# Attention with a relative-position bias, then two mixtures of experts: the bias stage and the attention in one program block

## The chip, the cores and the metric

The program runs on one core of one Trainium2 chip. The metric is the device time of one execution in microseconds (us), from start to end, with the inputs already in device memory. TensorE is called PE here, VectorE DVE, ScalarE ACT, GpSimd POOL and SyncE SP, as the profile does.

## The reference, cut to what matters

```python
# attention: q, k, v are [4, 8, 576, 64] (batch, heads, seq, dim)
scores = scale * q @ k^T
psi_rel = log1p(|i - j|);  psi_i = log1p(max(i, 1))
h = max((psi_rel / psi_i)[..., None] @ w1 + b1, 0)     # w1 [1, 32], b1 [32]
bias = h @ w2                                          # w2 [32, 8]: one 576x576 table a head
attn = softmax(scores + bias);  out = attn @ v
# then x [2304, 512] = out, heads side by side
# mixture 1: gate, softmax, one expert of 8 a token, h = relu(x @ w1[e]), h @ w2[e], times the gate
# mixture 2: h = max(x @ w1, x @ w2, x @ w3);  out = h @ w_out
```

All is float32. The change touches only the bias tables and the start of the attention. The two mixtures are as they were.

## The kernel before, in words

The kernel has three program blocks one after another, and each block has a stream of instructions for each engine. A block ends for all engines together.

**Bias stage** (`build_bias`, L53). It makes the eight 576x576 tables and stores them in device memory (`bias_table`, [row, head, column]). A step makes 16 rows for all heads. There are 36 steps, run as loops of 12 turns with 3 steps each (L148, L182, L124), with addresses from registers. In a step DVE makes three of four hidden tiles of 128x576 (L154, multiply and maximum) and ACT the fourth (L166, Relu). PE sums them with a block-diagonal w2 (L205, 8 matmuls of 288 columns into two banks), ACT evacuates the sums with a constant added (L174), and SP stores the result (L128, 288 KB). Hidden tiles, sums and evacuated tiles each have a ring of three. DVE's tiles for step s therefore wait for the sums of step s-3. ACT's evacuation of step s waits for the store of step s-3. On ACT the hidden tile of step s+2 stands ahead of the evacuation of step s.

Ahead of the loops SP issues the table of log distances (L116), w1 and b1 (L118) and four copies of w2 (L122). All of these raise one semaphore, `loaded`, for which DVE and PE wait. Then SP issues an identity and, for both units of head 0, the keys and queries (L443, L371, L372). ACT waits for DVE's `base` and then loads its function table. POOL sets some tiles to zero and issues 24 small loads for the later routing (L1072).

**Attention** (`build_attention`, L211). Eight heads, two units a head (a unit is two batches), five steps a unit. Ahead of the loop over heads the first unit is prepared, as a chain from engine to engine. PE transposes the keys and queries of unit (0, 0) (L652). ACT rounds them to the near part (L852, L854), and DVE makes the rest (L737, L738). PE transposes the 64 remaining rows (L669), DVE splits them (L746, L748), and POOL places them (L532, L534). Then PE makes the first scores (L598), DVE adds the bias and finds the maximum (L727), and ACT takes the exponential (L832). Here SP waits for all 36 stores, then loads the bias rows of head 0 (five tiles, L478 to L482), the values of both units (L406, L408) and the keys of head 1. In a step of the loop PE makes the scores of the next step, turns the probabilities of this one (L638), and multiplies them with the values of the unit before (L623).

**Mixtures** (`build_moe`, L1091): most of the time, untouched by the change.

The order in each engine's stream is written out by hand in the code. No planner sets it.

Of the kernel before, what the change touches and what calls it, by code (L numbers as in the profile page):

```python
# [16 lines left out]
ALU = mybir.AluOpType  # L17
# [35 lines left out]
def build_bias(nc, w1, b1, w2, bias_dram, stored, space, meanwhile_sync, meanwhile_gpsimd):  # L53
# [3 lines left out]

    G = P // HIDDEN
    ROWS = G * G
    STEPS = SEQ // ROWS
    WIN = 2 * SEQ - 1 - (G - 1)
    RING = len(stored)
# [12 lines left out]
    with ExitStack() as ctx:  # L78
        def sb(name, shape, dt=F32):
            return ctx.enter_context(nc.sbuf_tensor(name, shape, dt))  # L80

        def sem(name):
            return ctx.enter_context(nc.semaphore(name))

        both = sb("both", [P, WIN + SEQ // G])
        win, rows = both[:, 0:WIN], both[:, WIN:]
        scale = sb("scale", [P, SEQ // G])
        w1c = sb("w1c", [P, 1])
        b1c = sb("b1c", [P, 1])
        nb1 = sb("nb1", [P, 1])  # L90
        w2bd = sb("w2bd", [P, G * HEADS])
        hid = nc.alloc_sbuf_tensor_at("hid", [P, RING, G, SEQ], F32, offset=space)
        base = sb("base", [P, 1])
        staged = nc.alloc_sbuf_tensor_at("staged", [P, RING, SEQ], F32, offset=space + 4 * RING * G * SEQ)
        acc = ctx.enter_context(nc.psum_tensor("acc", [P, RING, 2, BANK], F32))
        cacc = ctx.enter_context(nc.psum_tensor("cacc", [P, BANK], F32))

        zeroed = sem("bias_zeroed")
        loaded = sem("bias_loaded")
        scales_done = sem("bias_scales_done")  # L100
        const_mm = sem("bias_const_mm")
        base_zeroed = sem("bias_base_zeroed")
        base_done = sem("bias_base_done")

        hid_dve = [sem(f"hidden_by_dve{r}") for r in range(RING)]
        hid_act = [sem(f"hidden_by_act{r}") for r in range(RING)]
        summed = [sem(f"bias_summed{r}") for r in range(RING)]
        evacuated = [sem(f"bias_evacuated{r}") for r in range(RING)]
        block = ctx.enter_context(nc.Block())
        rows_per_step = bias_dram.rearrange("(s r) h j -> s (r h) j", r=ROWS)  # L110
        TURNS = STEPS // RING
        LOADS = 16 * (3 + G)

        @block.sync
        def _(sp):
            sp.dma_start(both[:], tables_dram).then_inc(loaded, 16)  # L116
            for dst, src in ((w1c, w1), (b1c, b1.rearrange("(a k) -> a k", a=1))):
                sp.dma_start(dst[:], src.rearrange("a k -> k a").unsqueeze(0).broadcast_to([G, HIDDEN, 1])).then_inc(loaded, 16)  # L118

            sp.wait_ge(zeroed, 1)  # L120
            for g in range(G):
                sp.dma_start(w2bd[g * HIDDEN:(g + 1) * HIDDEN, g * HEADS:(g + 1) * HEADS], w2).then_inc(loaded, 16)  # L122
            meanwhile_sync(sp)
            with sp.Fori(0, TURNS) as t:  # L124
                for r in range(RING):

                    sp.wait_ge(evacuated[r], t + 1)
                    sp.dma_start(rows_per_step[bass.ds(t * RING + r, 1)].rearrange("a p j -> (a p) j"),  # L128
                                 staged[:, r, :]).then_inc(stored[r], 16)

        @block.gpsimd
        def _(pool):
            meanwhile_gpsimd(pool)

        @block.vector
        def _(dve):
            nc.vector.memset(w2bd[:], 0.0).then_inc(zeroed, 1)
            nc.vector.memset(base[:], 0.0).then_inc(base_zeroed, 1)
            dve.wait_ge(loaded, LOADS)
            nc.vector.tensor_scalar(nb1[:], b1c[:], -1.0, None, ALU.mult).then_inc(scales_done, 1)  # L140
            nc.vector.tensor_scalar(scale[:], rows, w1c[:], None, ALU.mult).then_inc(scales_done, 1)

            dve.wait_ge(const_mm, 1)
            dve.wait_ge(base_zeroed, 1)
            nc.vector.tensor_copy(base[0:DVE_Q * HIDDEN, :], cacc[0:DVE_Q * HIDDEN, 0:1]).then_inc(base_done, 1)
            dve.wait_ge(scales_done, 2)

            with dve.Fori(0, TURNS) as t:  # L148
                for r in range(RING):

                    dve.wait_ge(summed[r], t)
                    for q in range(DVE_Q):
                        u = (t * RING + r) * G + q
                        last = nc.vector.tensor_scalar(  # L154
                            hid[:, r, q, :], win[:, bass.ds(-G * u + (SEQ - G), SEQ)], scale[:, bass.ds(u, 1)],
                            nb1[:], ALU.mult, ALU.max)
                    last.then_inc(hid_dve[r], 1)

        @block.scalar
        def _(act):  # L160
            def hidden(t, r):

                act.wait_ge(summed[r], t)
                for q in range(DVE_Q, G):
                    u = (t * RING + r) * G + q
                    last = nc.scalar.activation(hid[:, r, q, :], win[:, bass.ds(-G * u + (SEQ - G), SEQ)], ACT.Relu,  # L166
                                                bias=b1c[:], scale=scale[:, bass.ds(u, 1)])
                last.then_inc(hid_act[r], 1)

            def evacuate(t, r):  # L170

                act.wait_ge(summed[r], t + 1)
                act.wait_ge(stored[r], 16 * t)
                nc.scalar.activation(staged[:, r, :].rearrange("p (a j) -> p a j", a=2), acc[:, r, :, 0:HALF],  # L174
                                     ACT.Identity, bias=base[:]).then_inc(evacuated[r], 1)

            act.wait_ge(scales_done, 2)
            act.wait_ge(base_done, 1)

            for r in range(RING - 1):  # L180
                hidden(0, r)
            with act.Fori(0, TURNS - 1) as t:  # L182
                for r in range(RING):
                    ahead = r + RING - 1
                    hidden(t + ahead // RING, ahead % RING)
                    evacuate(t, r)
            hidden(TURNS - 1, RING - 1)
            for r in range(RING):
                evacuate(TURNS - 1, r)

        @block.tensor
        def _(pe):
            pe.wait_ge(loaded, LOADS)
            for q in range(DVE_Q):
                last = nc.tensor.matmul(cacc[q * HIDDEN:(q + 1) * HIDDEN, 0:1], w2bd[:], b1c[:], start=True, stop=True)
            last.then_inc(const_mm, 1)
            with pe.Fori(0, TURNS) as t:
                for r in range(RING):

                    pe.wait_ge(hid_dve[r], t + 1)  # L200
# [1802 lines left out]
```

## Time and profile before

| what | value |
|---|---|
| median of 3 runs | 1037.75 us (1036.89 to 1039.24) |
| profiled execution, own time | 1038.5 us |
| its span | 1036.9 us |
| granted PE clock, mean | 0.981 |
| PE busy | 961.4 us, 93% of the span |
| DVE / ACT / POOL busy | 530.9 / 392.2 / 283.4 us |
| largest groups of PE | L1612 193.2, L1533 145.7, L1567 140.3, L638 80.7, L598 69.3 us |

The profile is of one execution. Its span runs from the first to the last instruction, and 1.6 us of its own time lie around it. Matmuls are pipelined, so a busy PE isn't PE at its peak. A time in the span is counted from its start: the bias stage fills the first 67 us, the attention reaches to about 370 us. An idle stretch of an engine is put down to what ended it.

### The profile page before, as it was taken

How to read it: one execution, taken by the hardware profiler on the slowest of the kernel's cores; microseconds unless marked ns; L12 is line 12 of the kernel's file. 1: busy time of each engine (PE TensorE's matmuls, PEld its weight loads, DVE VectorE, ACT ScalarE, POOL GpSimd, SP SyncE). 2: the span in 40 equal slices, each digit the busy share in tenths (PEclk: the TensorE clock that was granted, in tenths of full speed). 3: DMA queues.
4: the chain of work that ended last, by engine and by line, in shares of the span. 5: the costliest groups of instructions: out<-in, count | busy, mean ns of one | idle time of the engine just before them, and what ended most of it. 6: DMA issues, size and time to landing. Idle time of an engine off the chain costs nothing.

```text
span 1036.9 us, 19507 instructions
## 1 busy us (share of the span) xinstructions
PE 961.4 (93%) x6432; PEld 790.2 (76%) x6432; DVE 530.9 (51%) x1066; ACT 392.2 (38%) x810; POOL 283.4 (27%) x310
## 2 busy tenths in 40 slices
PE   4869999999999974799999999999999999999998
PEld 1227677677676663688888888888989999999997
DVE  6966666667566548444444457444352323333331
ACT  5967777777777652242100024034311010111100
POOL 5014150010101035796300059268531010100100
PEclk9989999999999996899999999999999999999999
DMA  7565544454443256775300036246411010100001
GB/s 168 203 205 133 128 125 110 110 119 106 100 114 85 76 163 205 237 211 172 104 21 21 22 122 210 84 131 186 132 51 41 21 41 21 41 21 11 21 11 31
DMA packets 125746, 106.68 MB, mean 103 GB/s; under 512 B 88073, under 2 KB 91305, under 8 KB 125689
## 3 DMA queue, kind: packets, MB, share of 16 engines
q1 hardware_dynamic: 86600, 56.27, 19.3%
q10 hardware_dynamic: 33632, 34.02, 11.6%
q0 software_dynamic: 5456, 15.60, 4.8%
q8 instruction: 40, 0.66, 0.3%
q14 instruction: 18, 0.14, 0.0%
HBM read 79.24 MB, written 26.61 MB: 102 GB/s over the span
## 4 chain that ended last, share of the span: by engine, by line
PE 56%; POOL 3%; issue 2%; DMA 1%; DVE 1%; ACT 1%; ACTq 0%; POOLq 0%
PE moe_banks L1612 19%; PE moe_banks L1533 12%; PE moe_banks L1567 12%; PE moe_banks L1629 7%; POOL slots L1301 3%; PE moe_banks L1551 2%; PE moe_banks L1518 1%; DMA x_tok<-in_moe_w_out 1%; PE moe_banks L1470 1%; PE moe_banks L1595 1%; PE moe_banks L1479 0%; DMA x_behind<-x_rows_by_tile,source 0%; POOL far_weights L1301 0%; ACT x_tok L1431 0%; POOL x_tok L1339 0%
## 5 line engine op out<-in xcount | busy, mean ns | idle before, releaser
L1612 PE MATMUL moe_banks<-yT,slots 128*128 128x384 f32 x1080 | 193.2, 334 | 0.7 <-ACT best L1439 0.7
L1612 PEld LDWEIGHTS moe_banks<-yT,slots 128*128 128x128 f32 x1080 | 187.9, 188 | 1.5 <-ACT best L1439 1.0
L1301 POOL TENSOR_TENSOR slots<-x_tok,slots 128x512 fp32r<-128x512 f32 (+1 forms) x116 | 140.9, 1249 | 155.3 <-ACT slots L1409 154.9
L1409 ACT CAST slots<-x_tok 128x512 fp32r<-128x512 f32 (+1 forms) x116 | 67.9, 602 | 261.9 <-PE moe_banks L1533 128.1
L1533 PE MATMUL moe_banks<-slots,xT 128*128 x600 | 145.7, 399 | 1.2 <-issue 1.2
L1567 PE MATMUL moe_banks<-slots,hT 128*128 x600 | 140.3, 389 | 0.8 <-POOL slots L1301 0.8
L727 DVE CUSTOM_DVE_ANT_0 probs<-s_ps,bias 128x576 f32<-128x576 f32 x144 | 103.7, 754 | 71.0 <-PE s_ps L598 51.4
L1533 PEld LDWEIGHTS moe_banks<-slots,xT 128*128 128x128 f32 x600 | 112.6, 191 | 25.0 <-issue 1.9
L1567 PEld LDWEIGHTS moe_banks<-slots,hT 128*128 128x128 f32 x600 | 112.6, 188 | 24.4 <-issue 1.1
L832 ACT ACTIVATE probs<-probs,negmax 128x576 f32<-128x576 f32 x144 | 110.6, 771 | 22.3 <-DVE negmax L727 21.6
L1867 DVE TENSOR_TENSOR best<-best,moe_banks 128x384 f32<-128x384 f32 x36 | 19.9, 554 | 132.8 <-PE moe_banks L1612 127.5
L840 ACT COPY pT<-t_ps 128x512 f32<-128x512 f32 x112 | 64.9, 581 | 60.4 <-PE t_ps L638 60.3
L638 PE MATMUL t_ps<-ident,probs 128*128 128x128 f32 x576 | 80.7, 281 | 3.7 <-ACT probs L832 1.1
L598 PE MATMUL s_ps<-kT,qT 64*128 64x288 f32 x768 | 69.3, 313 | 11.7 <-DVE negmax L727 9.0
L1629 PE MATMUL moe_banks<-wo,u 128*128 128x512 f32 x324 | 76.5, 393 | 0.0
L638 PEld LDWEIGHTS t_ps<-ident,probs 128*128 128x128 f32 x576 | 63.2, 142 | 16.0 <-issue 9.5
L598 PEld LDWEIGHTS s_ps<-kT,qT 64*128 64x128 f32 x768 | 54.4, 189 | 27.1 <-issue 15.3
L1439 ACT COPY best<-moe_banks 128x384 f32<-128x384 f32 x33 | 15.8, 478 | 152.4 <-PE moe_banks L1612 152.4
L623 PE MATMUL o_ps<-pT,v_raw 128*64 128x288 f32 x512 | 72.5, 415 | 0.7 <-ACT out_T L859 0.5
L1629 PEld LDWEIGHTS moe_banks<-wo,u 128*128 128x128 f32 x324 | 60.1, 188 | 12.2
L1347 POOL DMA_INDIRECT out<-o,out_row_of x15 | 14.7, 982 | 198.2 <-ACT o L1446 198.2
L532 POOL TENSOR_TENSOR kT<-last_T,one 128x128 fp32r<-128x128 f32 x32 | 14.6, 457 | 198.1 <-DVE last_T L748 198.1
(199 smaller groups left out, 1186.9 us busy)
## 6 DMA issues: line engine op xcount, KB each, us to landing
x_tok<-in_moe_w ACTq DMA_DIRECT2D x96, 256.0 KB
bias_table<-staged SPq DMA_DIRECT2D x36, 288.0 KB, 2.1
bias<-bias_table SPq DMA_DIRECT2D x32, 288.0 KB, 2.7
result_rows<-y SPq DMA_DIRECT2D x25, 256.0 KB, 2.0
x_tok<-in_moe_w ACTq DMA_DIRECT2D x24, 192.0 KB
k_raw<-in_k SPq DMA_DIRECT2D x32, 128.0 KB, 2.4
q_raw<-in_q SPq DMA_DIRECT2D x32, 128.0 KB, 2.5
v_raw<-in_v SPq DMA_DIRECT2D x32, 128.0 KB, 2.3
```

What stands on the lines that cost most here:

```text
L598: last = nc.tensor.matmul(s_ps[:, slot, half, 0:HALF], qT[u][a][lanes, s * P:(s + 1) * P], keys[c][lanes, at:at + HALF], start=(n == 0), s ...
L623: last = nc.tensor.matmul(o_ps[b * DH:(b + 1) * DH, 0:HALF], v_raw[u][:, b, jb, :], moving, start=(jb == 0), stop=(jb == FULL))
L638: last = nc.tensor.transpose(t_ps[:, bank, jb * P:(jb + 1) * P], probs[:, slot, at:at + P], ident[:])
L727: nc.vector.tensor_tensor_reduce(probs[:, step, b * SEQ:(b + 1) * SEQ].rearrange("p (a j) -> p a j", a=2), s_ps[:, slot, :, 0:HALF], bias[ ...
L832: nc.scalar.activation(row, row, ACT.Exp, bias=negmax[:, 2 * step + b:2 * step + b + 1], scale=-1.0, accum_out=sums[:, u, tile:tile + 1]). ...
L840: nc.scalar.copy(*turned_probs(u, s, b, bank)).then_inc(emptied[bank], 1)
L1301: nc.gpsimd.tensor_tensor(rest, raw(n, rows), near.bitcast(F32), ALU.subtract).then_inc(part_done(e, part)[0], 1)
L1409: nc.scalar.copy(near, raw(n, rows)).then_inc(near_done, 1)
L1533: return nc.tensor.matmul(h_ps[:, side, :], xT[t % 2][:, a, d * P:(d + 1) * P], weights(parity, b, d * FF + side * BANK), start=first, sto ...
L1567: last = nc.tensor.matmul(y_ps, hT[:, a, f * P:(f + 1) * P], weights(parity, b, 2 * PER_W + f * MODEL), start=(f == 0 and n == 0), stop=(f ...
L1612: last = nc.tensor.matmul(u_ps[m], final_weight(far, slots, m, d, a, f), yT[:, c, d, :], start=(d == 0 and k == 0), stop=(d == KD - 1 and ...
L1629: last = nc.tensor.matmul(o_ps[j], u[:, c, f, j * P:(j + 1) * P], wo[:, a, f, :], start=(f == 0 and k == 0), stop=(f == KF2 - 1 and k == 2))
```

## The change

The bias stage becomes four functions, one for each engine but POOL, that are called inside the attention's block. The loops become 36 steps written out, with constant addresses. After a step each engine runs a hook, `after_step`, in which parts of the attention's start are placed. The ring semaphores become counts over all steps.

- SP: w2's four copies are now issued by ACT. After the first loads SP issues the identity and the keys and queries of unit (0, 0), those of unit (0, 1) after the store of step 4, the values of unit (0, 0) after step 20 and of unit (0, 1) after step 22. Bias tiles 0 to 3 of head 0 are loaded after steps 9, 17, 25 and 33, the last after step 35.
- POOL: the routing loads wait for `loaded`. Its split work (L532, L534) follows in the same stream.
- ACT: one unused Relu of 128x1 ahead of the steps, so that the function table is loaded there. The near parts come after the evacuations of steps 10 and 11.
- DVE: the rests after steps 13 and 14, the last rows after step 19.
- PE: keys and queries turned after step 8, the last rows after step 16, the first scores after step 33. Sums go to the attention's own banks: in turn s_ps[0], s_ps[1] and the joined r_ps/o_ps, and the last three steps to t_ps, r_ps/o_ps, t_ps. PE waits for all 36 evacuations before it turns the first probabilities.

```diff
-def build_bias(nc, w1, b1, w2, bias_dram, stored, space, meanwhile_sync, meanwhile_gpsimd):
+def bias_stage(nc, sb, sem, w1, b1, w2, bias_dram, stored, space, banks, first_bank):
...
+    def sync(sp, after_step):
+        sp.dma_start(both[:], tables_dram).then_inc(loaded, 16)
+        for dst, src in ((w1c, w1), (b1c, b1.rearrange("(a k) -> a k", a=1))):
...
+        after_step(sp, -1)
+        for s in range(STEPS):
+            sp.wait_ge(evacuated, s + 1)
+            sp.dma_start(rows_per_step[s], staged[:, s % RING, :]).then_inc(stored[s % RING], 16)
+            after_step(sp, s)
...
+    def scalar(act, after_step):
+        act.wait_ge(zeroed, 1)
+        for g in range(G):
+            act.dma_start(w2bd[g * HIDDEN:(g + 1) * HIDDEN, g * HEADS:(g + 1) * HEADS], w2).then_inc(loaded, 16)
+        act.wait_ge(base_zeroed, 1)
+        nc.scalar.activation(unused[:], base[:], ACT.Relu).then_inc(base_zeroed, 1)
...
+            act.wait_ge(summed, s + 1)
+            if s >= RING:
+                act.wait_ge(stored[s % RING], 16 * (s // RING))
...
         def first_split(pool):
...
+            pool.wait_ge(*bias_sems["loaded"])
             routing["load"](pool)
...
+        LAST_SUMS = {BIAS_STEPS - 3: t_ps, BIAS_STEPS - 2: ro_ps, BIAS_STEPS - 1: t_ps}
...
+        TURN_AT, NEAR_AT, REST_AT, TURN_LAST_AT, LAST_AT = 8, (10, 11), (13, 14), 16, 19
+        SCORES_AT = BIAS_STEPS - 3
...
+            def after_step(sp, s):
+                if s == -1:
+                    sp.dma_start(ident[:], identity_dram).then_inc(ident_in, 16)
+                    keys_queries(sp, 0, 0)
+                if s == 4:
+                    keys_queries(sp, 0, 1)
+                if s == 20:
+                    sp.wait_ge(zeroed, 1)
+                    load_values(sp, 0, 0)
+                if s == 22:
+                    load_values(sp, 0, 1)
+                steps = s - 1
+                if steps > 0 and steps % (P // BIAS_ROWS) == 0 or s == BIAS_STEPS - 1:
+                    steps = SEQ // BIAS_ROWS if s == BIAS_STEPS - 1 else steps
+                    for r in range(BIAS_RING):
+                        sp.wait_ge(bias_stored[r], 16 * stored_by(r, steps))
+                    bias_tile(0, (steps - 1) // (P // BIAS_ROWS))
...
+                        if first and u == 0 and s == 0:
+                            pe.wait_ge(bias_sems["evacuated"], BIAS_STEPS)
...
+            def after_step(pe, s):
+                if s == TURN_AT:
+                    pe.wait_ge(ident_in, 16)
+                    pe.wait_ge(bias_sems["base_done"], 1)
+                    for g in (KEYS, QUERIES):
+                        bank, count = prologue_fill(g)
+                        turn_rows(0, 0, g, t_ps[:, bank]).then_inc(filled[bank], 1)
+                if s == TURN_LAST_AT:
+                    prepare_last(0, 0, prologue_fill(LAST))
+                if s == SCORES_AT:
+                    pe.wait_ge(zeroed, 1)
+                    pe.wait_ge(bias_sems["evacuated"], SCORES_AT - 1)
+                    scores(0, 0, 0, [prologue_fill(QUERIES)])
```

## Rows read from the trace of the kernel before

**Rows 1.** Stretches: busy us of each engine (count), granted PE clock, DMA share, GB/s.
```profile
15.00:50.00 35.00, 28.46 (x392) 10.36 (x388) 35.00 (x73) 34.72 (x49) 0.00 (x0) 1.00 0.53 200
70.65:74.85 4.20, 1.81 (x12) 1.46 (x12) 0.32 (x1) 0.00 (x0) 3.95 (x11) 0.50 0.99 310
72.40:80.00 7.60, 5.69 (x34) 5.02 (x35) 2.89 (x8) 2.62 (x6) 2.24 (x7) 0.50 0.73 183
80.00:92.00 12.00, 10.82 (x92) 8.52 (x90) 8.64 (x21) 9.94 (x24) 1.70 (x4) 0.99 0.60 141
```

**Rows 2.** Timeline, 0 to 60 us: start, us, engine, line, [idle before <-releaser].
```profile
1.98 0.56 SPq L118 DMA_DIRECT2D b1c<-in_b  x1
2.58 1.86 SPq L122 DMA_DIRECT2D w2bd<-in_w  x4
...
3.34 10.87 POOL L1072 DMA_DIRECT2D mod_id<-in_moe_modality_id  x20
...
9.60 0.59 SPq L371 DMA_DIRECT2D k_raw<-in_k  x1
9.82 0.15 DVE L140 TENSOR_SCALAR nb<-b1c 128x1 f32<-128x1 f32 x1 [8.90 <-DMA w2bd<-in_w]
...
10.46 1.28 ACT L166 ACT_TABLE_LOAD   x1 [10.46 <-DVE base L145]
...
10.85 49.46 DVE L154 TENSOR_SCALAR hid<-both,scale,nb 128x576 f32 x100 [0.48 <-DVE scale L141]
...
13.79 0.52 SPq L372 DMA_DIRECT2D rem_raw<-in_q  x1
...
24.70 0.75 ACT L174 ACTIVATE staged<-acc,base 128x576 f32<-128x576 f32 x1
...
26.08 0.75 ACT L174 ACTIVATE staged<-acc,base 128x576 f32<-128x576 f32 x1
```

**Rows 3.** DMA issues of 0 to 120 us: kind, count, KB each, median us to landing.
```profile
bias_table<-staged SPq DMA_DIRECT2D x36, 288.0 KB, 2.1
...
mod_id<-in_moe_modality_id POOLq DMA_DIRECT2D x16, 1.0 KB, 3.5
```

**Rows 4.** Timeline, 59 to 100 us: the end of the bias stage.
```profile
58.76 5.47 DVE L154 TENSOR_SCALAR hid<-both,scale,nb 128x576 f32 x11
...
61.77 0.86 ACT L166 ACTIVATE hid<-both,b1c,scale 128x576 f32<-128x576 f32 x1
...
64.29 1.18 PE L205 MATMUL acc<-hid,w2bd 128*32 128x288 f32 x16 [0.29 <-DVE hid L154]
65.54 0.74 ACT L174 ACTIVATE staged<-acc,base 128x576 f32<-128x576 f32 x1 [0.73 <-PE acc L205]
```

**Rows 5.** The same timeline: from the new block to the second exponential.
```profile
67.22 0.35 POOL L551 MEMSET own_batch<- 64x64 f32 x2 [52.25 <-POOLq L78]
...
68.69 0.69 DVE L737 TENSOR_TENSOR kT<-t_ps,kT 128x512 fp32r<-128x512 f32 x1 [4.46 <-ACT kT L852]
...
69.90 0.28 DVE L746 CAST last_T<-t_ps 128x128 fp32r<-128x128 f32 x1
...
74.53 0.76 DVE L727 CUSTOM_DVE_ANT_0 probs<-s_ps,bias 128x576 f32<-128x576 f32 x1 [4.03 <-PE s_ps L598]
...
75.33 0.78 ACT L832 ACTIVATE probs<-probs,negmax 128x576 f32<-128x576 f32 x1 [6.17 <-DVE negmax L727]
...
79.49 0.78 ACT L832 ACTIVATE probs<-probs,negmax 128x576 f32<-128x576 f32 x1
```

**Rows 6.** Instructions of L154, all, then of 12.8 to 15.3 us: ns min/median/max.
```profile
L154 DVE TENSOR_SCALAR hid<-both,scale,nb x108: 561/573/833, 10.9 to 63.7; 128x576 f32 x108
...
L154 DVE TENSOR_SCALAR hid<-both,scale,nb x6: 561/605/833, 12.3 to 15.2; 128x576 f32 x6
```

**Rows 7.** Timeline of POOL, then of DVE, around 753 us, and L1874's instructions.
```profile
750.10 6.81 POOL L1358 TENSOR_TENSOR wo<-x_tok,wo 128x3072 fp32r<-128x3072 f32 x1 [8.97 <-ACT wo L1455]
...
753.44 3.70 DVE L1874 CAST u<-best 128x384 fp32r<-128x384 f32 x1
...
L1874 DVE CAST u<-best x36: 359/359/3697, 733.6 to 1021.3; 128x384 fp32r<-128x384 f32 x36
```

More of the change, by code:

```diff
@@ L76, in build_bias @@
     tables_dram = nc.inline_tensor(np.ascontiguousarray(tables), name="bias_tables").ap()
[L78 to L193, printed above, removed]
-            for q in range(DVE_Q):
[L195 to L200, printed above, removed]
-                    pe.wait_ge(hid_act[r], t + 1)
-                    pe.wait_ge(evacuated[r], t)
-                    for a in range(2):
-                        for q in range(G):
-                            last = nc.tensor.matmul(acc[q * HIDDEN:(q + 1) * HIDDEN, r, a, 0:HALF], w2bd[:],
-                                                    hid[:, r, q, a * HALF:(a + 1) * HALF], start=True, stop=True)
-                    last.then_inc(summed[r], 1)
@@ new lines, in scalar, with hidden, evacuate @@
+    def scalar(act, after_step):
[4 more added lines that the diff above has]
+        nc.scalar.activation(unused[:], base[:], ACT.Relu).then_inc(base_zeroed, 1)
+        def hidden(s):
+            if s >= RING:
+                act.wait_ge(summed, s - RING + 1)
+            for q in range(DVE_Q, G):
+                u = s * G + q
+                last = nc.scalar.activation(hid[:, s % RING, q, :], window(u), ACT.Relu, bias=b1c[:], scale=scale[:, u:u + 1])
+            last.then_inc(hid_act, 1)
+        def evacuate(s):
+            act.wait_ge(summed, s + 1)
+            if s >= RING:
+                act.wait_ge(stored[s % RING], 16 * (s // RING))
+            nc.scalar.activation(staged[:, s % RING, :].rearrange("p (a j) -> p a j", a=2), banks(s)[:, :, 0:HALF],
+                                 ACT.Identity, bias=base[:]).then_inc(evacuated, 1)
+        act.wait_ge(scales_done, 2)
+        act.wait_ge(base_done, 1)
+        for s in range(RING - 1):
+            hidden(s)
+        for s in range(STEPS):
+            if s + RING - 1 < STEPS:
+                hidden(s + RING - 1)
+            evacuate(s)
+            after_step(act, s)
@@ new lines, in tensor @@
+    def tensor(pe, before_step, after_step):
+        pe.wait_ge(loaded, LOADS)
+        for q in range(DVE_Q):
+            last = nc.tensor.matmul(first_bank[q * HIDDEN:(q + 1) * HIDDEN, 0:1], w2bd[:], b1c[:], start=True, stop=True)
+        last.then_inc(const_mm, 1)
+        for s in range(STEPS):
+            pe.wait_ge(hid_dve, s + 1)
+            pe.wait_ge(hid_act, s + 1)
+            before_step(pe, s)
+            for a in range(2):
+                for q in range(G):
+                    last = nc.tensor.matmul(banks(s)[q * HIDDEN:(q + 1) * HIDDEN, a, 0:HALF], w2bd[:],
+                                            hid[:, s % RING, q, a * HALF:(a + 1) * HALF], start=True, stop=True)
+            last.then_inc(summed, 1)
+            after_step(pe, s)
@@ L490, in values_rows @@
+            bias_sync(sp, after_step)
             def values_rows(it):
```

140 lines of the change are left out of this document (92 added, 48 removed).

## The prediction

> **What bounds the kernel now.** I read the stretches first, then the timeline of the first 100 us. In 15 to 50 us DVE is busy for all 35.00 us, PE for 28.5, at full clock [rows 1]: DVE bounds the bias stage. Its first hidden tile starts at 10.85 and the last ends at 58.76 + 5.47 = 64.23 [rows 2, 4]. That is 53.38 us for 108 tiles, 0.494 each and 1.48 a step, without a gap. Then comes the hand-over: the last sums start at 64.29, the last evacuation at 65.54 [rows 4], the new block at 67.22, the first bias addition at 74.53, the first exponential at 75.33 and that of the second step at 79.49 [rows 5]. From DVE's last tile to the first exponential are 11.1 us in which PE runs its few matmuls at a granted 0.50, and it keeps that level, 1.2 GHz, to 80 us. From 80 on it has 0.99, 2.4 GHz [rows 1]. After that the attention runs as a steady chain, in which nothing is tied to the start of the program, only to what came before. So what moves the second exponential moves the end by as much. I follow that one point.
>
> **Part 1, the loads ahead of the stage.** DVE starts at 9.82, released by w2's copies. SP issues these from 2.58 to 4.44, behind b1, while POOL issues its loads from before 3.34 [rows 2]. In the new order ACT issues the copies beside SP's first loads, and POOL's loads wait for `loaded`. The last needed issue is then b1's, from 1.98 on. Its landing under a full queue isn't shown. From below it is the 2.1 us of a store, from above the whole 9.82. The nearest row is POOL's small loads in the same microseconds, 3.5 us [rows 3], which gives 1.98 + 0.56 + 3.5 = 6.0. I take 6.1 (4.6 to 9.8): 3.7 us earlier. DVE's first hidden tile stays 1.03 behind it (10.85 - 9.82), at 7.1. ACT's table load of 1.28 goes from after `base` to this wait. It lay beside DVE's first tiles, so it brings nothing on DVE's path, only ACT starts level with DVE.
>
> **Part 2, steps written out.** The register instructions of the loops run on the sequencers while the tiles run, and DVE has no gap [rows 1, 2]. I take 0 for their going. If an address cost DVE anything, the gain would be up to 0.03 a tile, 3 us. The nearest row, a stage without any gap, says 0.
>
> **Part 3, DVE's moved work.** The rests of keys and queries start 0.61 after each other, and the last rows take from 69.90 to the start of POOL's part at about 70.65, with two waits of DVE for itself: 0.8. Sum 2 x 0.61 + 0.8 = 2.0 us [rows 1, 5]. DVE is the bound, so all is on the path. 7.1 + 53.4 + 2.0 = 62.5.
>
> **Part 4, what SP does between the stores.** The keys and queries of unit (0, 1) are eight issues. In the trace such a group goes from 9.60 to 14.31, 4.7 us [rows 2]. After step 4's store they stand ahead of step 5's store. That one lands 0.4 + 4.7 + 2.1 = 7.2 us after step 4's evacuation ends, and 8.2 if the queue holds it up by 1 us beside the small packets. ACT's evacuation of step 8 needs it. ACT would be there after 4 x 1.38 - 0.62 = 4.9 us (24.70 to 26.08 is a step at ACT's own pace [rows 2]). So ACT is 3.3 us late. The two near copies after steps 10 and 11 add 1.2. Of these 4.5 us some are covered. ACT's hidden tile is ahead of DVE's: the last one ends at 62.6, 1.6 before DVE's [rows 4], and I take 1.0 at step 8. The ring lets DVE go on for 1.6 more: it needs sums of 65.5 only two steps after its tiles [rows 4]. Left are 1.9 us (0.7 to 3.4). The other moved loads, values of 2.2 us after steps 20 and 22 and bias tiles of 0.9, are shorter than the ring's 4.4 us less a landing of 2.1. I take 0. Likewise PE's nine transposes: PE has 35.0 - 28.5 free in 35 us [rows 1], 0.3 a step. 64.4.
>
> **Part 5, POOL's work beside DVE.** The splitting and the routing bias, 3.95 us in 11 instructions [rows 1], and two memsets of 0.35 [rows 5] ran while DVE stood nearly still. Now they run beside the hidden tiles. The trace has one clear place for this: POOL's subtraction runs from 750.10 to 756.91, and a DVE cast from SBUF to SBUF, which takes 359 ns elsewhere, starts at 753.44 and ends at 757.14, just behind it [rows 7]. DVE stood still until POOL was done. The hidden tiles are of that sort: 576 columns in 0.494 us, while 512 columns out of PSUM take 0.69 [rows 5, 6]. Bounds: 0 if the two interleave, 4.3 if each POOL instruction stops DVE for its length. I take 3.3, three quarters, as POOL waits for itself in between. POOL's descriptor writing costs less: the six tiles beside its last loads have a median of 605 ns against 573, and one has 833 [rows 6]. Over a longer stretch, early, partly inside the stall of part 4: 0.3. Together 3.6: DVE's last tile ends at 68.0.
> The Trainium skill says in "GPSIMD Engine Reference", section "Key points", that POOL shares its SBUF interfaces with DVE and contends with DVE instructions in a two-port mode or with two SBUF inputs. "VectorE: DVE Perf Modes", section "Mode 2×_2P", counts a float32 multiply by a scalar from SBUF to SBUF into that mode. By that rule the place where POOL's work was, beside an idle DVE, was the good one, and the change gives up to 4.3 us back. Without the rule the same sum would come out 3.6 us lower.
>
> **Part 6, the new hand-over.** Bias addition and first scores are ready: DVE adds right behind its last tile, 0.76 for the first half. ACT is last. Sums start 0.06 after DVE's end, evacuation 1.25 later, and it holds ACT for 0.63 [rows 4]. The score matmuls after step 33, about 1.1 us at full clock, exceed PE's free time of the last two steps by 0.2. So the first exponential comes 2.1 behind DVE: 70.1, against 75.33. The next step also comes sooner: in the trace 79.49 - 75.33 = 4.2 us, with PE at 0.50 and scores only begun behind the exponential. With PE at full clock and the second scores made while ACT still evacuates, what is left is two exponentials of 0.77 and the copy of the first probabilities, about 2.3 us: 1.9 less (1.0 to 2.3). What is late next is that copy.
>
> **Sum.** 75.33 - 70.1 = 5.2, plus 1.9: 7.1 us. Against the profiled execution: span 1036.9 - 7.1 = 1029.8, own time 1038.5 - 7.1 = 1031.4. The median of the runs shown lies 0.75 below that execution, so I predict 1037.75 - 7.1 = 1030.6.
>
> **The rivals.** *A, POOL and DVE don't hinder each other.* For it: the tiles beside POOL's loads are only 32 ns longer in the median [rows 6]. Against: rows 7. It gives 3.6 more: 1027.0. If the loads also end at 5 us, 1026.
> *B, the loads come no sooner.* `loaded` has seven parts, and the keys of unit (0, 0) are now issued 2 us earlier, beside them. For it: loads alone fill the queues to 0.99 in 70.65 to 74.85 [rows 1]. Against: POOL's loads are gone. It costs the 3.7 of part 1: 1034.3.
> *C, slower: the ring of stores decides every step.* An evacuation waits for the store three steps back. Three steps are 4.4 us, of which evacuation and issue take about 1, so from a landing of 3.4 to 3.5 us on the ring sets the pace, and each further us costs 36 / 3 = 12 us. The stage now loads about 2.6 MB of keys, values and bias rows between its stores. Stores land in 2.1 us at a DMA share of 0.53 [rows 1, 3]. For a loss the landing would have to be over 4.1 us all along. At 4.6 the time is 1030.6 + 13 = 1044. It speaks against it that the extra bytes are a quarter of the stores' 10.4 MB (36 x 288 KB) and come in seven short bursts.
> *D, the time comes back later.* Were the attention paced by weight loads or POOL's early chunks, nothing would reach the end: 1037.8. But these are issued behind the same chain.
>
> **How the numbers follow.** Forecast 0.60, with its own range 1028.3 to 1033.0 (part 4 at either end, part 1 a microsecond or so to either side). A 0.20, B 0.13, C 0.03, D 0.04. The range reaches to A and to B: 1026.3 to 1034.5. Beyond it lie C, D and a joint of the worst parts. About 0.2% (2 us) is what a measurement of this kernel can tell from no change. Faster 0.93 (forecast, A, B), the same 0.04 (D), slower 0.03 (C).
>
> **What would show it.** `loaded` near 6 us and DVE's first tile near 7. A gap of DVE of about 2 us around steps 12 to 15, ended by PE, with ACT's evacuation of step 8 released by a store. Tiles of DVE of 0.8 to 1 us beside POOL's placing, around 40 to 50 us, 573 ns elsewhere. The first exponential near 70 and the second step's 2.3 later, PE at 1.00 throughout. From there to the end the length as before, within 1 us. I am wrong if DVE's tiles are longer throughout, if DVE waits for PE in most steps (C), or if the stretch from the second exponential to the end changes.

## The result and the profile after

| | runs | median us | range |
|---|---|---|---|
| before | 4 | 1037.49 | 1036.89 to 1039.24 |
| after | 4 | 1026.55 | 1024.52 to 1028.92 |

The ratio is 0.9893, with an interval of 0.9868 to 0.9917: 10.9 us faster. Forecast were 1030.6 us and a gain of 7.1. The direction and the place were right, the size fell short by nearly 4 us: 1026.55 lies below the forecast's own range (1028.3 to 1033.0) and 0.25 us inside the wide one, which reached that far for rival A. The profiled execution of the kernel after took 1028.92 us, its span is 1027.1.

The busy times of the page: TensorE still fills nearly the whole span.

```profile
PE 962.7 (94%) x6432; PEld 791.8 (77%) x6432; DVE 532.9 (52%) x1066; ACT 391.0 (38%) x811; POOL 286.0 (28%) x310
...
bias_table<-staged SPq DMA_DIRECT2D x36, 288.0 KB, 2.4
```

The timeline of the kernel after, from its start to the second exponential (columns as in [rows 2]); it answers to [rows 2, 4, 5]:

```profile
0.93 1.81 ACTq L131 DMA_DIRECT2D w2bd<-in_w  x4
...
6.17 0.15 DVE L112 TENSOR_SCALAR nb<-b1c 128x1 f32<-128x1 f32 x1 [5.26 <-DMA w2bd<-in_w]
...
6.60 21.93 DVE L124 TENSOR_SCALAR hid<-both,scale,nb 128x576 f32<-128x576 f32 x42
...
8.38 10.71 POOL L1098 DMA_DIRECT2D mod_id<-in_moe_modality_id  x20
...
20.00 0.74 ACT L147 ACTIVATE staged<-s_ps,base 128x576 f32<-128x576 f32 x1 [1.04 <-DMA bias_table<-staged]
...
22.34 4.93 SPq L105 DMA_DIRECT2D bias_table<-staged  x5
...
24.79 0.74 ACT L147 ACTIVATE staged<-ro_ps,base 128x576 f32<-128x576 f32 x1 [1.91 <-DMA bias_table<-staged]
...
28.81 0.69 DVE L754 TENSOR_TENSOR kT<-t_ps,kT 128x512 fp32r<-128x512 f32 x1 [0.28 <-ACT kT L874]
...
39.59 24.66 DVE L124 TENSOR_SCALAR hid<-both,scale,nb 128x576 f32<-128x576 f32 x48 [0.15 <-DVE last_T L765]
...
40.04 0.67 POOL L527 TENSOR_TENSOR qz<-last_T,own_batch 128x128 fp32r<-128x128 f32 x1
...
64.17 0.74 DVE L744 CUSTOM_DVE_ANT_0 probs<-s_ps,bias 128x576 f32<-128x576 f32 x1
...
65.95 0.74 ACT L147 ACTIVATE staged<-t_ps,base 128x576 f32<-128x576 f32 x1 [0.50 <-PE t_ps L171]
66.58 0.77 ACT L854 ACTIVATE probs<-probs,negmax 128x576 f32<-128x576 f32 x1
...
68.73 0.78 ACT L854 ACTIVATE probs<-probs,negmax 128x576 f32<-128x576 f32 x1
```

Three distances are to be read here. DVE's first hidden tile starts at 6.60, 4.25 us sooner than before. Its last ends at 39.59 + 24.66 = 64.25, the same place as the 64.23 of before: the moved work and POOL's work have used up the earlier start. From there to the first exponential it is 2.33 us instead of 11.1, and to the second 4.48 instead of 15.3. So the second exponential comes 79.49 - 68.73 = 10.76 us sooner.

The stretches of the kernel after (columns as in [rows 1]):

```profile
15.00:50.00 35.00, 25.76 (x353) 10.21 (x349) 34.53 (x69) 31.02 (x45) 11.74 (x22) 1.00 0.71 228
66.58:68.73 2.15, 1.32 (x14) 0.91 (x11) 1.44 (x4) 2.10 (x6) 0.00 (x0) 1.00 0.37 129
...
362.00:366.00 4.00, 4.00 (x21) 4.00 (x20) 1.86 (x3) 2.24 (x5) 3.02 (x3) 0.52 0.20 66
```

DVE is still the full engine of the bias stage, POOL now works 11.74 us beside it, and at the hand-over TensorE keeps its full 2.4 GHz, where it had 0.50 before, from 70.65 to 80 us [rows 1]. The last row lies at the other end of the attention, where the mixtures begin. There 32 transposes come first. TensorE's timeline in the kernel before, after, and before once more:

```profile
371.68 3.69 PE L1470 MATMUL moe_banks<-ident_late,x_tok 128*128 128x128 f32 x32 [2.00 <-PEq L221]
```
```profile
359.80 6.64 PE L1496 MATMUL moe_banks<-ident_late,x_tok 128*128 128x128 f32 x32 [2.00 <-PEq L194]
```
```profile
372.10 6.59 PE L1470 MATMUL moe_banks<-ident_late,x_tok 128*128 128x128 f32 x32 [2.00 <-PEq L221]
```

The attention ends 371.68 - 359.80 = 11.88 us sooner. The profiled spans differ by only 9.8, since in the execution after the clock fell to 0.52 for a part of the transposes, which cost 2.95. The kernel before does the same in its second profile. A third length, 5.0 to 5.35 us, is found in most of the other profiles. So it comes with either kernel. The same holds of a wait of TensorE some 40 to 50 us on: 9.04 us before and 8.01 after in this first pair, 4.7 to 7.0 in the four profiles of the third group of experiments, and 1.3 to 1.6 in the eight of the first two groups, the second one of the kernel before among them. It goes with the group, and so with the chip or the time, and not with the change. So I measure the change at the start of the mixtures where one trace stands for a kernel, and by medians where there are several runs.

### The profile page after: what moved, and what is told of

Same layout as the page of the kernel before. It is cut to its first block, busy times and chain, and to the rows that moved or that the text cites. A ratio compares the mean times of both kernels' runs of the same rounds, so it can differ in the third digit from the quotient of the medians.

```text
span 1027.1 us, 18990 instructions
## 1 busy us (share of the span) xinstructions
PE 962.7 (94%) x6432; PEld 791.8 (77%) x6432; DVE 532.9 (52%) x1066; ACT 391.0 (38%) x811; POOL 286.0 (28%) x310
## 4 chain that ended last, share of the span: by engine, by line
PE 59%; POOL 2%; DVE 2%; issue 1%; ACT 0%; ACTq 0%
PE moe_banks L1638 22%; PE moe_banks L1559 13%; PE moe_banks L1593 12%; PE moe_banks L1655 7%; PE moe_banks L1577 2%; POOL slots L1327 2%; PE moe_banks L1496 1%; PE moe_banks L1544 1%; PE moe_banks L1621 1%; PE moe_banks L1505 0%; DVE slots L1802 0%; POOL x_tok L1365 0%; DVE in_lane L1740 0%; ACT x_tok L1457 0%; ACT slots L1435 0%
## 5 line engine op out<-in xcount | busy, mean ns | idle before, releaser
L617 PE MATMUL ro_ps<-pT,v_raw 128*64 128x288 f32 x512 | 72.5, 415 | 0.7 <-ACT out_T L881 0.5
```

The costliest lines, as they stand in the source:

```text
L617: last = nc.tensor.matmul(o_ps[b * DH:(b + 1) * DH, 0:HALF], v_raw[u][:, b, jb, :], moving, start=(jb == 0), stop=(jb == FULL))
```

## The experiments

All are compared with runs of the kernel before on the same chip: median 1035.52 us (22 runs) in the first group of four, 1035.12 (9 runs) in the second group, 1036.9 (one run) in the third.

### The same kernel again (after_again)

No edit.

> The changed kernel once more, beside the kernel before. Theory 1 (the change is worth 10.8 us at the second step's exponential and 11.9 us at the end of the attention; the 3.0 us lost behind it in the first profile are a matter of the moment at which PE's clock is lowered): here the second step's exponential starts again at 68.7 us, and the 32 first transposes of the mixtures take either 3.7 or up to 6.7 us, with the span longer or shorter by just that. Theory 2 (the change itself causes the slow transposes): they take 6.6 us again. Time 1025 to 1029 us, 0.9875 to 0.991 of before.

Measured: 1023.14 us, ratio 0.9882 (0.9866 to 0.9898). First hidden tile 7.07, last one's end near 64.9, second exponential 69.19, the first 32 transposes 5.24. Of the gain of 12.4 us 11.4 to 11.8 are there at the start of the mixtures (360.32 against 371.68 and 372.10). The first profile's 2.95 us extra at these transposes were 1.55 here (5.24 - 3.69), so their length isn't fixed by the kernel.

### One block, but the preparation behind the stage (prep_behind)

The main lines of the edit:

```
-        TURN_AT, NEAR_AT, REST_AT, TURN_LAST_AT, LAST_AT = 8, (10, 11), (13, 14), 16, 19
-        SCORES_AT = BIAS_STEPS - 3
+        TURN_AT, TURN_LAST_AT, LAST_AT, SCORES_AT = [BIAS_STEPS - 1] * 4
```

> One block, steps written out, loads as in the changed kernel, but the first unit's preparation (turning, rounding, splitting, placing, first scores) stands behind step 35 on every engine. Theory 1 (most of the hand-over's 11.1 us was the preparation as a chain, the end of the block only about 1.5 us of it): DVE's last tile ends about 2.3 us sooner than in the changed kernel (near 62), the first exponential comes about 8 to 9 us behind it (near 71) and the second step's near 75, so 6 us of the gain are lost: 1032 to 1033 us. Theory 2 (the barrier between the blocks was the main cost): the first exponential near 68 and 1028 us.

Measured: 1033.19 us, ratio 0.9975 (0.9966 to 0.9984). Timeline of DVE and ACT at the hand-over:

```profile
62.08 1.56 DVE L124 TENSOR_SCALAR hid<-both,scale,nb 128x576 f32<-128x576 f32 x3 [0.45 <-PE ro_ps L171]
69.03 0.69 DVE L749 TENSOR_TENSOR kT<-t_ps,kT 128x512 fp32r<-128x512 f32 x1 [5.40 <-ACT kT L868]
...
75.00 0.76 DVE L739 CUSTOM_DVE_ANT_0 probs<-s_ps,bias 128x576 f32<-128x576 f32 x1 [4.15 <-PE s_ps L591]
...
66.91 0.74 ACT L147 ACTIVATE staged<-t_ps,base 128x576 f32<-128x576 f32 x1 [0.65 <-PE t_ps L171]
...
75.80 0.77 ACT L848 ACTIVATE probs<-probs,negmax 128x576 f32<-128x576 f32 x1 [6.30 <-DVE negmax L739]
...
79.97 0.78 ACT L848 ACTIVATE probs<-probs,negmax 128x576 f32<-128x576 f32 x1
```

The two exponentials come at 75.80 and 79.97, where the kernel before has them at 75.33 and 79.49. My expectation, 71 and 75, was wrong. The earlier loads gave 4.3 us at the front. But DVE waits for the ring: it stands behind step 13 for 1.0 us and behind steps 29, 31 and 34 for 0.4 to 0.6, each time until TensorE has made sums, while ACT waits for stores six times in this stage, 5.8 us in all. With POOL's loads beside it the stage takes 57.07 us and not 53.38, and its last tile ends only 0.6 us sooner. The last sums start 2.0 us behind that tile, 0.06 in the kernel before [rows 4]. From there the preparation runs one engine after the other as in the kernel before, with TensorE at 0.50 from 72 to 80 us.

The end of the block has a price of its own, which this run hides behind those late sums. From the end of ACT's last evacuation to the first transpose it is 1.13 us in the kernel before (65.54 + 0.74 to 67.41) and 0.10 here (66.91 + 0.74 to 67.75). TensorE's timeline, before and in this run:

```profile
67.41 0.63 PE L652 MATMUL t_ps<-ident,k_raw 128*128 128x128 f32 x4 [1.94 <-PEq L78]
```
```profile
67.75 0.63 PE L645 MATMUL t_ps<-ident,k_raw 128*128 128x128 f32 x4 [0.90 <-issue]
```

So one block and the early loads alone bring the second exponential no sooner. The 10.8 us there need the preparation to lie beside the stage, and the early loads pay for its room.

### The kernel before with its steps written out (steps_written_out)

The four loops over the turns of the ring become Python loops, nothing else. One of them:

```
-            with dve.Fori(0, TURNS) as t:
+            for t in range(TURNS):
```

> The kernel before with nothing changed but its four loops of the bias stage, which are written out with constant addresses. Theory 1 (register instructions are hidden, as predicted): DVE's tiles start 0.489 us after each other as before, first tile 0.2 to 0.4 us sooner as no registers are set up, time within 0.5 us of before (1037). Theory 2 (addresses from registers cost DVE up to 0.03 us a tile): 3 us faster.

Measured: 1032.40 us, ratio 0.9972 (0.9961 to 0.9982). The tiles start 0.489 us after each other as before, so within the stage the forecast of nothing holds. Yet the kernel is 3.1 us faster, a miss. The trace shows 1.1 to 1.5 us of it at the attention's end (its last exponential starts at 358.69, against 359.79 and 360.21): 0.4 to 0.7 are there by the second exponential, the rest is a head loop of 36.07 us a head instead of 36.20. The remainder lies behind the start of the mixtures, where executions differ anyway. But the 3.1 us stand between medians of 11 and 22 runs, and the interval is clear of 1. prep_behind, whose steps are written out too, looks the same: 2.3 us faster by medians, with its second exponential no sooner and the mixtures only 0.4 to 0.9 us sooner (371.25 against 371.68 and 372.10). So of the whole change's 12.4 us in after_again up to 3 may come from writing the steps out, and only 1.1 to 1.5 of these are seen in a trace. The kernel before wasn't profiled in this group, so where the rest lies isn't settled.

### POOL's routing loads and routing bias later (pool_all_later)

```
-            pool.wait_ge(*bias_sems["loaded"])
-            routing["load"](pool)
...
+            place_last(0, 1)
+            routing["load"](pool)
             token_bias(pool)
-            place_last(0, 1)
```

> The changed kernel with POOL's routing loads and routing bias behind the placing of unit (0, 1), so that in the bias stage POOL only places unit (0, 0). Theory 1 (POOL's work makes the hidden tiles beside it longer, by 1.3 us in all beside its descriptor writing and 1.1 us beside its elementwise work, but the first part hides a wait of DVE for ACT's near copy, which is late by the stores): no tile of DVE over 0.50 us except four beside the placing, DVE waits about 1.6 us for the near copy at step 13 in place of 0.3, and its last tile ends 0.8 us sooner (63.4); time 0.5 to 1 us below the changed kernel. Theory 2 (ACT isn't late enough to matter): the tile ends 2.1 us sooner, at 62.1, and the time is 2 us lower.

Measured: 1023.66 us, ratio 0.9891 (0.9869 to 0.9914): as the kernel after. DVE's tiles are back at 0.489 from the start and only the placing stretches some, by 0.73 us in all. 42 tiles take 20.64 us where they took 21.93, so POOL's loads had cost 1.3. The last tile ends at 63.48, as expected. The gain to the first exponential is 0.9 us (65.67). Head 0 then takes 34.85 us instead of 32.95 and gives 1.9 back. DVE's timeline shows why it brought so little, a wait that had been 0.28:

```profile
28.47 0.69 DVE L753 TENSOR_TENSOR kT<-t_ps,kT 128x512 fp32r<-128x512 f32 x1 [1.29 <-ACT kT L873]
```

### The kernel before again (before_again)

No edit.

> The kernel before, profiled beside the others. Theory 1 (the wait of 8 to 9 us some 40 us into the mixtures, seen in both first profiles and in none of the second series, belongs to the chip or the moment and not to a kernel): it isn't there, and the span from the end of the attention is 660 to 662 us as in the second series; the second step's exponential starts at 79.5 us and a head of the attention's loop takes 36.20 us. Theory 2 (the kernels with written-out steps lose that wait by themselves): it is there.

Measured: 1036.37 us. Second exponential 79.84, heads of 36.20, first transposes 6.59, and 1.3 us where the first profile had its 9.04. The attention's numbers repeat to 0.4 us, the mixtures' first 50 us don't.

### Second unit's keys and queries ahead of the stage (keys_up_front)

```
                 if s == -1:
                     sp.dma_start(ident[:], identity_dram).then_inc(ident_in, 16)
                     keys_queries(sp, 0, 0)
-                if s == 4:
                     keys_queries(sp, 0, 1)
```

> The changed kernel with the keys and queries of unit (0, 1) issued right behind those of unit (0, 0), not between the stores of steps 4 and 5. Theory 1 (the late stores cost 0.3 to 0.6 us only, because POOL's work had slowed DVE's tiles by then): ACT waits for no store at steps 8, 10 or 11, DVE doesn't wait for the near copy at step 13, and DVE's last tile ends 0.3 to 0.6 us sooner, at 63.7; time within 1 us of the changed kernel. Theory 2 (as predicted, the stores cost 1.9 us): it ends at 62.3 and the time is 2 us lower.

Measured: 1021.15 us, ratio 0.9868 (0.985 to 0.9885). SP has no eight issues between two stores any more, the wait at step 13 is gone, and DVE's last tile ends near 63.85, as the first theory expected. ACT still waits for stores twice, 1.4 us in all, where it had four times and 5.0. `loaded` is there at 6.23, within the 6.10 to 6.64 of the other profiles with these first loads and POOL's behind them. Second exponential 68.20. The kernel after has no runs in this group. Against the kernel before of its group this one gains 14.0 us where after_again gained 12.4, and the two intervals overlap.

### Routing loads and bias behind head 2 (routing_after_head2)

The two calls of pool_all_later, put behind the written-out heads, ahead of the loop over heads.

> The changed kernel with POOL's routing loads and routing bias behind head 2's placing, where POOL has nothing else. Theory 1: DVE's last tile ends at 63.5 as with the same work behind unit (0, 1), and now the 1.9 us that were lost there in head 0 (unit (1, 0) placed late) are kept: the ninth step's exponentials and all later ones 1.0 us ahead of the changed kernel, time 1 us lower. Theory 2 (POOL's loads disturb DVE wherever they are): the gain is lost again within the attention.

Measured: 1023.51 us, ratio 0.9886 (0.9866 to 0.9905). Head 0 loses nothing here (the second step's exponential at 69.15, the second head's first at 99.99). But the stage ends at 64.93 instead of the 63.5 expected. The timeline of ACT and DVE has the reason:

```profile
25.91 0.74 ACT L147 ACTIVATE staged<-ro_ps,base 128x576 f32<-128x576 f32 x1 [3.70 <-DMA bias_table<-staged]
...
29.93 0.69 DVE L753 TENSOR_TENSOR kT<-t_ps,kT 128x512 fp32r<-128x512 f32 x1 [2.74 <-ACT kT L873]
```

The store held up behind SP's eight issues landed still later, and DVE stood 2.74 us. This is part 4 of the forecast, at the size that I gave it and above. pool_all_later has the same instructions in this stage and waited 1.29, so the size goes by the execution. In the kernel after, POOL's loads had slowed DVE by 1.3 us by the time it would have waited, and 0.28 were left (0.51 in after_again).

### Both (keys_and_routing)

> Both: keys and queries of unit (0, 1) up front, routing behind head 2. Theory 1 (the near copy's wait of 1.3 us, which shows once POOL doesn't slow DVE, comes from the late stores): DVE's last tile ends at 62.2, the first exponential starts at 64.4, all 2.2 us ahead of the changed kernel; time 2 us lower. Theory 2 (something else makes ACT late): the wait stays, and the times are those of the routing moved alone.

Measured: **1019.61 us** (1017.66 to 1020.03), ratio 0.9848 (0.9831 to 0.9864), the lowest median here (its interval overlaps that of keys_up_front), 15.5 us below the kernel before. DVE's timeline:

```profile
6.91 20.65 DVE L124 TENSOR_SCALAR hid<-both,scale,nb 128x576 f32<-128x576 f32 x42
27.48 0.68 DVE L752 TENSOR_TENSOR kT<-t_ps,kT 128x512 fp32r<-128x512 f32 x1
...
38.24 24.23 DVE L124 TENSOR_SCALAR hid<-both,scale,nb 128x576 f32<-128x576 f32 x48
62.40 0.74 DVE L742 CUSTOM_DVE_ANT_0 probs<-s_ps,bias 128x576 f32<-128x576 f32 x1
```

No wait ahead of the rests, 42 tiles in 20.65 us and not in 21.93, and the second exponential at 66.69. DVE's first hidden tile starts at other times in these runs (6.54 to 7.07), so I count the second exponential from it:

| kernel | from DVE's first hidden tile to the second exponential, us |
|---|---|
| after, after_again | 62.13, 62.12 |
| keys_up_front | 61.53 |
| pool_all_later, routing_after_head2 | 61.27, 62.61 |
| keys_and_routing | 59.78 |

The keys' edit alone gains 0.6 us. The routing's edit alone gains 0.9 or loses 0.5, as the store lands. Together they gain 2.3. POOL's loads and the late stores are two delays that lie beside each other: with one gone, the other takes its place. The transposes took 3.69 us in this profile, so its own time may flatter it by a microsecond or two; the attention's end at 346.01 (347.91 before the two edits) doesn't depend on that.

### Which of the load edits brought the early start (w2_on_sp, pool_loads_early)

w2_on_sp issues w2's four copies from SP behind b1, as before the change. pool_loads_early takes away the wait that holds POOL's loads back:

```
-            pool.wait_ge(*bias_sems["loaded"])
             routing["load"](pool)
```

> The changed kernel with w2's four copies issued by SP again, behind b1 (POOL's routing loads still wait). Theory 1 (most of the earlier start comes from the place of w2's copies, 1.9 us of issues behind b1): DVE's first instruction behind the loads starts about 2 us later than in the changed kernel's 6.2, near 8.0. Theory 2 (it comes from POOL's loads being out of the way): it stays within 0.7 us, under 7.

> The changed kernel without POOL's wait for the loads: routing loads from 1.5 us on, as before the change (w2's copies stay with ACT). Theory 1 (the place of w2's copies is the main part): DVE starts near 7, under 1 us later than in the changed kernel, and its tiles are longer only up to about 15 us instead of 19.7. Theory 2 (POOL's loads in the queues are the main part): near 8.5.

Measured: 1028.01 and 1029.89 us. DVE's release in each:

```profile
7.21 0.15 DVE L115 TENSOR_SCALAR nb<-b1c 128x1 f32<-128x1 f32 x1 [6.30 <-DMA w2bd<-in_w]
```
```profile
8.60 0.15 DVE L112 TENSOR_SCALAR nb<-b1c 128x1 f32<-128x1 f32 x1 [7.69 <-DMA w2bd<-in_w]
```

From 6.17 it is 1.0 us later with w2 on SP and 2.4 later with POOL's loads early. With both as before it had been 3.65 [rows 2]. These are single runs: with the loads of the kernel after, the profiles have 6.10 to 6.64, and with those of the kernel before 9.19 to 10.04. So the order of the three cases is clear, their differences are good to about half a microsecond. POOL's loads in the first microseconds cost more than the place of w2's issue. By what way they delay w2's landing isn't shown.

### Only DVE's steps written out (dve_steps_written_out)

The edit of steps_written_out on DVE's loop alone.

> The kernel before with only DVE's loop of the bias stage written out. The attention's loop takes 36.20 us a head in both profiles of the kernel before and 36.07 in every kernel with all four loops written out; the difference is one DVE instruction, which starts 0.12 us later behind its semaphore. Theory 1 (it depends on where DVE's own instructions lie): 36.07 here. Theory 2 (it comes from another engine's stream): 36.20.

Measured: 1036.9 us, like the kernel before it. Yet a head takes 36.07 us, and the attention's last exponential starts at 358.39. All profiles of kernels with DVE's steps written out have this pace, and both of the kernel before have 36.20. So the pace of heads that start tens of microseconds later goes by the form of DVE's program ahead of them, and the other engines' loops can stay. Its own time doesn't show it: the mixtures took 665.0 us in this execution, with a wait of 6.41, against 660.0 in steps_written_out, and the kernel before wasn't profiled in this group.

### One long POOL instruction beside the tiles (one_long_pool_op)

keys_and_routing, with this behind the placing (`spare` is a new tile of 128x1024, which POOL fills ahead of it):

```
+            nc.gpsimd.tensor_tensor(spare[:], spare[:], spare[:], ALU.mult)
```

> The fastest kernel so far (keys up front, routing behind head 2) with one more POOL instruction behind the placing of unit (0, 0): a float32 multiply of a spare 128x1024 tile with itself, about 2.4 us alone, beside DVE's hidden tiles. Theory 1 (POOL and DVE take turns in small pieces, as the placing shows: 0.73 us more on DVE in 2.7 us of POOL): DVE's tiles beside it are of 0.6 to 0.75 us, 0.7 to 1.2 us more in all. Theory 2 (a long POOL instruction holds DVE's tile until it is done, as at 753 us before): one tile of over 2 us, DVE's last tile 2 us or more later.

Measured: 1026.53 us. POOL's instruction, then DVE's tiles of 38 to 46 us (ns min/median/max, first and last start):

```profile
40.28 2.11 POOL L549 TENSOR_TENSOR spare<-spare 128x1024 f32<-128x1024 f32 x1
```
```profile
L124 DVE TENSOR_SCALAR hid<-both,scale,nb x12: 569/572/2148, 37.9 to 45.6; 128x576 f32<-128x576 f32 x12
```

One tile took 2148 ns: it started 0.27 us behind POOL's instruction and ended 0.3 behind its end, as the cast of [rows 7] had. In both places where a long POOL instruction met a DVE tile, it held the tile until its own end. The short ones stretch the tiles beside them by 0.12 to 0.24 us each. DVE's last tile ends at 63.89 and not at 62.47, 1.4 us later (1.7 counted from its first one), a little under the 2 of the second theory. The first exponential came 4.7 us late (69.21), though: besides the 1.6 of this tile, ACT's last evacuation waited 2.31 us for a store. How the one brought about the other I did not follow up.

## Why the prediction was right, and where its sizes were off

The sum, term by term, each at the execution profiled:

| term | forecast us | measured us |
|---|---|---|
| first hidden tile (part 1) | 7.1 | 6.60 |
| tiles and steps (part 2) | 53.4 | 52.8, and 0.57 (what the kernel before lost beside POOL's loads) |
| DVE's moved work (part 3) | 2.0 | 2.0 |
| behind the stores (part 4) | 1.9 | 0.28 |
| beside POOL (part 5), more than before | 3.6 | 1.3 + 1.07 - 0.57 = 1.8 |
| DVE's last tile ends | 68.0 | 64.25 |
| to the first exponential (part 6) | 2.1 | 2.33 |
| to the second | 2.3 | 2.15 |
| gain at the second exponential | 7.1 | 10.76 |

**Parts 1, 3 and 6 held.** `loaded` came at 6.17 (6.1 forecast), though not by the load that part 1 named: the last issue was that of w2's copies on ACT, which ended at 0.93 + 1.81 = 2.74, and not b1's, and they released DVE. That the sum hit within 0.1 us is in part luck. The first hidden tile came 0.43 behind it and not 1.03. By part 6 most of the gain was to come at the hand-over, and it did. prep_behind confirms it: put the preparation back, and the second exponential is back at 79.97. One reading of the kernel before was wrong: in its profile TensorE had a granted 1.00 for its transposes up to 70 us and fell to 0.50 only then, so the low clock lay under the first scores and not under the whole hand-over.

**Part 4: mechanism right, place on the path wrong.** ACT waited for stores four times, 5.0 us in all:

```profile
ACT staged L147 <- DMA bias_table<-staged: 5.0, 4, 1.9
```

The longest is that of step 8's evacuation, as forecast, behind SP's eight issues from 17.13 to 22.30. With the 1.04 us at step 6 ACT was 2.95 us late by then, where the forecast had 3.3. DVE felt 0.28, not 1.9, and ACT's near copy ended it. In routing_after_head2 it felt 2.74 and in pool_all_later 1.29, both within the forecast's range of 0.7 to 3.4 for the delay alone. keys_up_front takes it away at its cause, and nothing remains at step 13.

**Part 5: two sizes off, in opposite directions.** This is the largest miss. The durations of DVE's tiles (ns min/median/max, first and last start), beside POOL's descriptor writing, beside its placing and routing bias, and with POOL idle:

```profile
L124 DVE TENSOR_SCALAR hid<-both,scale,nb x23: 572/608/639, 7.1 to 18.8; 128x576 f32<-128x576 f32 x23
...
L124 DVE TENSOR_SCALAR hid<-both,scale,nb x11: 568/689/801, 39.6 to 45.4; 128x576 f32<-128x576 f32 x11
...
L124 DVE TENSOR_SCALAR hid<-both,scale,nb x30: 565/568/570, 49.5 to 63.7; 128x576 f32<-128x576 f32 x30
```

Beside the placing and the routing bias the excess over 0.489 from start to start sums to 1.07 us. I had taken 3.3 from [rows 7]. That row tells the truth of a POOL instruction of 6.8 us, as one_long_pool_op tells it of one of 2.1, but POOL's pieces here are of 0.45 to 0.67 us. Its multiplications get longer themselves (0.45 us for the first, 0.67 for the three beside the tiles), so the two engines share the delay. The contention that the Trainium skill describes ("GPSIMD Engine Reference", section "Key points") is there. The page gives no size, and the trace has 1.07 us, a quarter of the bound of 4.3 that I had from the rows.

Not every POOL instruction costs DVE something. POOL's timeline, and DVE's tiles beside its two casts and the two instructions of L367:

```profile
41.29 0.67 POOL L527 TENSOR_TENSOR qz<-last_T,own_batch 128x128 fp32r<-128x128 f32 x1
41.91 0.52 POOL L365 CAST before_half<-const 128x128 f16<-128x128 f32 x1
42.38 0.54 POOL L365 CAST ones_half<-const 128x128 f16<-128x128 f32 x1
42.90 0.96 POOL L367 TENSOR_SCALAR is_mod<-mod_id 128x18 f32<-128x18 int32 x2
43.94 1.19 POOL L371 TENSOR_TENSOR bias_of<-is_mod,mod_bias 128x144 f32<-128x144 f32 x2
```
```profile
L124 DVE TENSOR_SCALAR hid<-both,scale,nb x4: 568/569/570, 42.2 to 43.7; 128x576 f32<-128x576 f32 x4
```

These four tiles are as short as with POOL idle. All of the 1.07 us lie beside POOL's seven TENSOR_TENSOR instructions: 0.65 beside the four of the placing, 0.42 beside the three of the routing bias, and nothing beside the four others. after_again, keys_up_front and w2_on_sp repeat it to 0.01 us a tile. Whether it is the two inputs, the types or the sizes that make the difference was not tried.

The descriptor writing cost 1.3 us and not 0.3 + 0.57: the median of the few tiles was right (605 ns then, 608 now), but POOL's loads now lie beside 23 tiles and not 6, and one tile of 907 ns came at their end.

**Where the sum failed.** The mechanisms of the forecast were there, and two of its terms were mis-sized. The larger is part 5's elementwise work: 3.3 us forecast, 1.07 measured. It comes 10 us behind the wait of step 13, so it adds in full, and only its price was wrong, read from one POOL instruction of 6.8 us. The other is part 4's 1.9 us, of which DVE felt 0.28. It was added to POOL's descriptor writing, and the two are parallel: a DVE that POOL has slowed by 1.3 us comes later to the place where it would wait for ACT, and finds the wait used up. The forecast saw that overlap and booked it as a small price of the descriptor writing (0.3) beside a full stall, while the trace has 1.3 of writing and 0.28 of stall. keys_up_front, routing_after_head2 and their joint run show that these two cover each other.

**Part 2 and "the length as before, within 1 us".** Within the stage written-out steps brought nothing, as forecast. But the attention from the second exponential to its last one took 279.18 us instead of 280.30: 1.1 us, just outside what I had allowed, and dve_steps_written_out puts it on the form of DVE's program. From the second exponential to the end of the span it took 958.4 instead of 957.4, and 952.2 in after_again against 955.0 in before_again, so in the mixtures the length as before holds only to several microseconds.

**The rivals.** A (no hindrance, 1027.0) has the nearest time, but not for its reason: hindrance there is, 2.4 us in all. It comes near because the 1.9 us that it keeps for part 4 stand in for 0.28 there and 1.8 beside POOL. B is refuted by `loaded`, C by the stores' median landing of 2.4 us (2.1 before) with DVE waiting for TensorE in no step, D by the start of the mixtures, 11.88 us sooner. What did come back, 2.95 us at the transposes, goes by the execution and not by the kernel.

## What to carry to other kernels

Before two delays are added, ask whether the second still finds its victim on time: where one slows an engine ahead of the point where the other would make it wait, about the larger one counts, and removing either alone shows much less than removing both. When work is hidden beside a bound stage, make the room first (here 4.3 us of earlier start for a stage that grew by 4.3 us) and keep long issue trains out from between the stores that a ring waits for. Take the price of two engines' contention from instructions of the length that will really meet, and of their kind, not from the longest one in the trace.

## What the hardware showed that I had not expected

- POOL's elementwise work beside back-to-back tiles of DVE: tiles of 0.489 us from start to start became 0.61 to 0.72 beside its TENSOR_TENSOR instructions, and POOL's 0.45 us became 0.67. Beside its casts and TENSOR_SCALARs of 0.5 us the tiles stayed at 0.49. One POOL instruction of 2.11 us held one tile for 2.15.
- The order of small loads is worth microseconds: the same w2 copies release DVE at 6.10 to 6.64, 7.21, 8.60 or 9.19 to 10.04 us, by where they are issued and by whether POOL's loads are issued beside them.
- TensorE's clock fell to 0.50 to 0.52 during the first transposes of the mixtures in some executions, of either kernel, and those 32 took 3.69, 5.0 to 5.35 or 6.6 us. What decides it isn't settled. Neither is what makes the wait of 1.3 to 9 us behind it, which goes with the chip or the time.
- Heads whose instructions are the same took 36.20 or 36.07 us a head, by the form of DVE's program ahead of it. The cause below that was not looked into.
